# Expert tiles of 124 rows in place of 128, in a fused attention and mixture-of-experts kernel

## The reference

```python
def _moe_ref(x, w_gate, w_noise, noise, w1, w2):    # x 2304 x 512, 8 experts, w1 512 x 1024, w2 1024 x 512
    logits = x @ w_gate
    noisy_logits = logits + np.log1p(np.exp(x @ w_noise)) * noise
    top2 = np.argpartition(-noisy_logits, 2, axis=1)[:, :2]
    ...
    for e in range(E):
        for k in range(2):
            mask = top2[:, k] == e
            h = np.maximum(x[mask] @ w1[e], 0.0)
            out[mask] += top2_w[mask, k, None] * (h @ w2[e])
```

## Time and profile before

| | us |
|---|---|
| median of 3 runs | 809.34 |
| lowest and highest | 808.65, 811.51 |
| the profiled execution | 808.09 |
| its span, first to last instruction | 805.9 |
| TensorE busy in it | 764.0 (95%) |
| VectorE, ScalarE, GpSimd busy | 496.5, 391.5, 383.5 |

### The profile page before, as it was taken

One profiled execution on the slowest core, in us unless ns is written; L12 is line 12 of the kernel. 1 busy time (PEld: TensorE's weight loads), 2 busy tenths in 40 slices (PEclk: granted clock), 3 DMA queues, 4 the chain that ended last, 5 costly groups with the idle time before them and its releaser, 6 DMA issues.

```text
span 805.9 us, 18520 instructions
## 1 busy us (share of the span) xinstructions
PE 764.0 (95%) x6658; PEld 623.0 (77%) x6658; DVE 496.5 (62%) x1233; ACT 391.5 (49%) x835; POOL 383.5 (48%) x440
## 2 busy tenths in 40 slices
PE   4886999999999998998999999999999999999995
PEld 2345676776776665978898998998998988988984
DVE  5997999998998897875436235235344344353311
ACT  5995888888888776515324133233232232241200
POOL 0007999899899784055334324324414413423312
PEclk9997999999999999999999999999999999999998
DMA  7786343353353373228623714804804705714213
GB/s 161 215 235 138 107 133 103 104 163 105 105 160 103 88 223 132 69 53 289 192 111 66 205 71 75 242 24 78 261 6 77 257 13 82 245 26 65 41 22 44
DMA packets 51576, 98.49 MB, mean 122 GB/s; under 512 B 12721, under 2 KB 21553, under 8 KB 51505
## 3 DMA queue, kind: packets, MB, share of 16 engines
q1 hardware_dynamic: 39920, 74.55, 30.4%
q0 software_dynamic: 10720, 22.72, 14.9%
q10 hardware_dynamic: 864, 0.29, 0.2%
HBM read 66.38 MB, written 20.53 MB: 108 GB/s over the span
## 4 chain that ended last, share of the span: by engine, by line
PE 51%; DMA 3%; issue 1%; POOL 0%; POOLq 0%; ACT 0%; DVE 0%; ACTq 0%; DVEq 0%
PE ps L765 26%; PE po L779 23%; DMA out_rows<-ys,iscat 2%; PE pt L601 2%; DMA xg<-x_rows,rowi 1%; POOL out_rows L1585 0%; POOLq L163 0%; ACT xT L1458 0%; POOL wrow L1577 0%; DVE ys L1247 0%; ACTq L1490 0%; POOLq L1582 0%; POOLq L1585 0%; POOLq L1583 0%; POOLq L1584 0%
## 5 line engine op out<-in xcount | busy, mean ns | idle before, releaser
L765 PE MATMUL ps<-xT,whi 128*128 128x320 f32 (+1 forms) x960 | 164.1, 309 | 1.6 <-ACT xT L1458 1.6
L779 PE MATMUL po<-whi,hT 128*128 128x512 f32 x640 | 159.9, 395 | 0.0
L765 PEld LDWEIGHTS ps<-xT,whi 128*128 128x128 f32 x960 | 145.6, 189 | 2.6 <-issue 1.1
L1469 ACT ACTIVATE hT<-ps 128x320 fp32r<-128x320 f32 x112 | 49.0, 437 | 200.6 <-PE ps L765 200.6
L1232 DVE SCALAR_TENSOR_TENSOR hT<-ps,hT 128x320 fp32r<-128x320 f32 x112 | 55.1, 492 | 137.6 <-ACT hT L1469 137.6
L779 PEld LDWEIGHTS po<-whi,hT 128*128 128x128 f32 x640 | 118.3, 188 | 24.5 <-DVE hT L1077 0.5
L1532 POOL TENSOR_SCALAR work<-work,rcp 128x576 f32<-128x576 f32 (+1 forms) x160 | 117.6, 745 | 24.9 <-DVE rcp L947 24.1
L934 DVE CUSTOM_DVE_ANT_0 ns<-ps,slab 128x576 f32<-128x576 f32 (+1 forms) x160 | 119.8, 750 | 10.1 <-PE ps L595 6.3
L1324 ACT ACTIVATE work<-ns,nmax 128x576 f32<-128x576 f32 (+1 forms) x160 | 123.1, 769 | 4.4 <-DVE nmax L934 4.3
L1572 POOL DMA_INDIRECT xg<-x_rows,igath x38 | 42.3, 1112 | 168.7 <-DVE ys L1247 76.9
L1585 POOL DMA_INDIRECT out_rows<-ys,iscat x35 | 58.9, 1682 | 101.1 <-DMA out_rows<-ys,iscat 68.8
(11 more groups left out here) (184 smaller groups left out, 1111.0 us busy)
## 6 DMA issues: line engine op xcount, KB each, us to landing
wraw<-in_mw SPq DMA_DIRECT2D x64, 512.0 KB, 9.9
slab<-work SPq DMA_DIRECT2D x36, 288.0 KB, 3.8
qraw<-in_qT SPq DMA_DIRECT2D x64, 144.0 KB, 2.9
vs<-in_v SPq DMA_DIRECT2D x32, 160.0 KB, 2.5
out_rows<-zeros SPq DMA_DIRECT2D x32, 152.0 KB
kraw<-in_kT SPq DMA_DIRECT2D x64, 72.0 KB, 2.5
x_rows<-xnat SPq DMA_DIRECT2D x8, 576.0 KB, 4.2
xg<-x_rows,igath POOLq DMA_INDIRECT x38, 3.7
```

The lines of the kernel that those rows point to most:

```text
L765: mm = nc.tensor.matmul(ps[n % 4 // 2][:, n % 2, 0:w], w1s[i][pw][:, c, f * P:(f + 1) * P], x[px][:, c, :], start=j == 0 and c == 0, stop= ...
L779: mm = nc.tensor.matmul(po[:, (i + t) % 2, :], hT[px][:, c, t * P:(t + 1) * P], w2s[i][pw][:, c, :], start=j == 0 and c == 0, stop=j == 2 ...
```

## The change

A tile now holds ROWS = 124 rows and a block 620. Half a block is 310 columns; in the first block the halves are 372 and 248. Transposes, their copies, the indirect DMAs and the scaling work on 124 rows. The second layer still loads 128 columns of `hT` as its stationary operand, the last four of which belong to the next tile and give rows of `po` that nobody reads; `hT` is declared flat for it. Where there are no such columns (the last `c` of the last tile, and the third tile of the first block) it loads 124. The number of the tile is found by multiplying with 1/124 and rounding by adding and subtracting a large constant, the lane by subtracting 124 times the tile; `colv` holds tile numbers in place of multiples of 128. The thresholds of the block count are scaled by 124/128. Its core (the early forms `xtr0`, `xcopy0`, `xlow0`, `hhigh0`, `hlow0` and `scaled0`, and `xlow` and `weights`, change in the same way as those shown; `hC` takes the place of `hT` where ReLU and the low part are written):

```diff
@@ -49,14 +49,16 @@
-BLK = BT * P
+ROWS = P - 4
+BLK = BT * ROWS
 HB = BLK // 2
...
 XB = 3
 XLATE = {2: 3, 4: 4}
-HA = XB * P
+HA = XB * ROWS
+MAGIC = 1.5 * 2 ** 23
...
-            hT = [tmp(f"hT{i}", [P, CF, BLK], F32R) for i in range(2)]
+            hT = [tmp(f"hT{i}", [P, CF * BLK], F32R) for i in range(2)]
+            hC = [h[:, :].rearrange("p (c t) -> p c t", c=CF) for h in hT]
...
                 for c in range(CD):
-                    mm = tr(pt[i][:, c * P:(c + 1) * P], xg[t][:, c * P:(c + 1) * P], P)
+                    mm = tr(pt[i][:, c * ROWS:(c + 1) * ROWS], xg[t][0:ROWS, c * P:(c + 1) * P], ROWS)
                 mm.then_inc(xg_taken, 1)
...
-            def second(i, t, fresh=None):
+            def second(i, t, fresh=None, edge=False):
...
-                        mm = nc.tensor.matmul(po[:, (i + t) % 2, :], hT[px][:, c, t * P:(t + 1) * P],
+                        at, m = c * BLK + t * ROWS, ROWS if edge or (t == BT - 1 and c == CF - 1) else P
+                        mm = nc.tensor.matmul(po[0:m, (i + t) % 2, :], hT[px][:, at:at + m],
                                               w2s[i][pw][:, c, :],
...
-                second(0, t, CF if t == 0 else None)
+                second(0, t, CF if t == 0 else None, t == XB - 1)
...
+            def to_tile(which):
+                after(V.tensor_scalar(near[:, which], posk[:, which], 1.0 / ROWS, 0.5 / ROWS - 0.5, ALU.mult, ALU.add))
+                after(V.tensor_scalar(tileq[:, which], near[:, which], MAGIC, None, ALU.add))
+                after(V.tensor_scalar(hcol[:, which], tileq[:, which], -MAGIC, None, ALU.add))
+
+            def tile_and_lane(which):
+                to_tile(which)
+                after(V.scalar_tensor_tensor(out=lof[:, which], in0=hcol[:, which], scalar=float(-ROWS), in1=posk[:, which],
+                                             op0=ALU.mult, op1=ALU.add))
...
-            after(V.tensor_copy(poski[:, early], posk[:, early]))
-            after(V.tensor_scalar(loi[:, early], poski[:, early], P - 1, None, ALU.bitwise_and))
-            after(V.tensor_copy(lof[:, early], loi[:, early]))
-            after(V.tensor_tensor(hcol[:, early], posk[:, early], lof[:, early], ALU.subtract))
+            tile_and_lane(early)
...
-            after(V.tensor_tensor(over[:, :, :], inc[:, :, NT - 1:NT].broadcast_to([P, NE, NTHR]),
-                                  thr[:, 0:NT:BT].rearrange("p (a t) -> p a t", a=1).broadcast_to([P, NE, NTHR]),
-                                  ALU.is_gt))
+            after(V.scalar_tensor_tensor(out=over[:, :, :], in0=thr[:, 0:NT:BT].rearrange("p (a t) -> p a t", a=1)
+                                         .broadcast_to([P, NE, NTHR]), scalar=ROWS / P,
+                                         in1=inc[:, :, NT - 1:NT].broadcast_to([P, NE, NTHR]),
+                                         op0=ALU.mult, op1=ALU.is_lt))
...
-            after(V.tensor_copy(poski[:, :], posk[:, :]))
-            after(V.tensor_scalar(loi[:, :], poski[:, :], P - 1, None, ALU.bitwise_and))
-            after(V.tensor_copy(lof[:, :], loi[:, :]))
-            after(V.tensor_tensor(hcol[:, :], posk[:, :], lof[:, :], ALU.subtract))
+            tile_and_lane(slice(0, 2 * NT))
...
-                    V.tensor_scalar(ys[(i + t) % 2][:, :], po[:, (i + t) % 2, :], wrow[:, t, bass.ds(e, 1)], None, ALU.mult)\
+                    V.tensor_scalar(ys[(i + t) % 2][0:ROWS, :], po[0:ROWS, (i + t) % 2, :], wrow[0:ROWS, t, bass.ds(e, 1)], None, ALU.mult)\
                         .then_inc(y_done, 1)
...
-                nc.scalar.activation(xT[0][:, :, t * P:(t + 1) * P], pt[i][:, :].rearrange("p (c t) -> p c t", c=CD),
+                nc.scalar.activation(xT[0][:, :, t * ROWS:(t + 1) * ROWS],
+                                     pt[i][:, 0:CD * ROWS].rearrange("p (c t) -> p c t", c=CD),
                                      ACT.Copy).then_inc(xhi_done, 1)
...
-                nc.gpsimd.tensor_scalar(colv[:, :], iota[:, 0:NL], float(P), None, ALU.mult).then_inc(consts_done, 1)
+                nc.gpsimd.tensor_copy(colv[:, :], iota[:, 0:NL]).then_inc(consts_done, 1)
...
-                nc.gpsimd.indirect_dma_start(out=xg[t][:, :], out_offset=None, in_=xs[0:n, :],
-                                             in_offset=bass.IndirectOffsetOnAxis(ap=rows, axis=0),
+                nc.gpsimd.indirect_dma_start(out=xg[t][0:ROWS, :], out_offset=None, in_=xs[0:n, :],
+                                             in_offset=bass.IndirectOffsetOnAxis(ap=rows[0:ROWS], axis=0),
...
-                nc.gpsimd.indirect_dma_start(out=out, out_offset=bass.IndirectOffsetOnAxis(ap=index, axis=0),
-                                             in_=ys[i][:, :], in_offset=None, compute_op=ALU.add,
+                nc.gpsimd.indirect_dma_start(out=out, out_offset=bass.IndirectOffsetOnAxis(ap=index[0:ROWS], axis=0),
+                                             in_=ys[i][0:ROWS, :], in_offset=None, compute_op=ALU.add,
```

More of the change, by code:

```diff
@@ L276, in build @@
         posk = cut([P, 2 * NT])
-        poski = cut([P, 2 * NT], I32)
-        loi = cut([P, 2 * NT], I32)
+        near = cut([P, 2 * NT])
+        tileq = cut([P, 2 * NT])
         over = cut([P, NE, len(range(0, NT, BT))])
@@ L750, in xtr0 @@
                 for c in range(CD):
-                    mm = tr(dst[:, c * P:(c + 1) * P], xg[t][:, c * P:(c + 1) * P], P)
+                    mm = tr(dst[:, c * ROWS:(c + 1) * ROWS], xg[t][0:ROWS, c * P:(c + 1) * P], ROWS)
                 mm.then_inc(xg_taken, 1)
@@ L1076, in hlow0 @@
                 dve.wait_ge(hhi_done, n + 1)
-                V.scalar_tensor_tensor(out=hT[1][:, f, cols], in0=ps[n % 4 // 2][:, n % 2, 0:cols.stop - cols.start], scalar=0.0,
-                                       in1=hT[0][:, f, cols].bitcast(F32), op0=ALU.max, op1=ALU.subtract)\
+                V.scalar_tensor_tensor(out=hC[1][:, f, cols], in0=ps[n % 4 // 2][:, n % 2, 0:cols.stop - cols.start], scalar=0.0,
+                                       in1=hC[0][:, f, cols].bitcast(F32), op0=ALU.max, op1=ALU.subtract)\
                     .then_inc(hlo_done, 1)
@@ L1084, in scaled0 @@
                 dve.wait_ge(y_added, C_ADD + 16 * (t - 1))
-                V.tensor_scalar(ys[t % 2][:, :], po[:, t % 2, :], wrow[:, t, 0:1], None, ALU.mult).then_inc(y_done, 1)
+                V.tensor_scalar(ys[t % 2][0:ROWS, :], po[0:ROWS, t % 2, :], wrow[0:ROWS, t, 0:1], None, ALU.mult).then_inc(y_done, 1)
             evac0(TILES - 7)
@@ L1221, in xlow @@
                 dve.wait_ge(xhi_done, g + 1)
-                cols = slice(t * P, (t + 1) * P)
-                V.tensor_tensor(xT[1][:, :, cols], pt[i][:, :].rearrange("p (c t) -> p c t", c=CD),
+                cols = slice(t * ROWS, (t + 1) * ROWS)
+                V.tensor_tensor(xT[1][:, :, cols], pt[i][:, 0:CD * ROWS].rearrange("p (c t) -> p c t", c=CD),
                                 xT[0][:, :, cols].bitcast(F32), ALU.subtract).then_inc(xlo_done, 1)
@@ L1231, in block_of @@
                     dve.wait_ge(hhi_done, C_HALVES * b + n + 1)
-                    V.scalar_tensor_tensor(out=hT[1][:, f, cols], in0=ps[n % 4 // 2][:, n % 2, 0:HB], scalar=0.0,
-                                           in1=hT[0][:, f, cols].bitcast(F32), op0=ALU.max, op1=ALU.subtract)\
+                    V.scalar_tensor_tensor(out=hC[1][:, f, cols], in0=ps[n % 4 // 2][:, n % 2, 0:HB], scalar=0.0,
+                                           in1=hC[0][:, f, cols].bitcast(F32), op0=ALU.max, op1=ALU.subtract)\
                         .then_inc(hlo_done, 1)
@@ L1399, in xcopy0 @@
                 act.wait_ge(xg_taken, t + 1)
-                nc.scalar.activation(xTa[0][:, :, t * P:(t + 1) * P], src.rearrange("p (c t) -> p c t", c=CD),
+                nc.scalar.activation(xTa[0][:, :, t * ROWS:(t + 1) * ROWS],
+                                     src[:, 0:CD * ROWS].rearrange("p (c t) -> p c t", c=CD),
                                      ACT.Copy).then_inc(xhi_done, 1)
@@ L1406, in hhigh0 @@
                 act.wait_ge(h_ready, n + 1)
-                nc.scalar.activation(hT[0][:, f, cols], ps[n % 4 // 2][:, n % 2, 0:cols.stop - cols.start], ACT.Relu)\
+                nc.scalar.activation(hC[0][:, f, cols], ps[n % 4 // 2][:, n % 2, 0:cols.stop - cols.start], ACT.Relu)\
                     .then_inc(hhi_done, 1)
@@ L1412, in scaled0 @@
                 act.wait_ge(w_rows, 16 * XB)
-                nc.scalar.activation(ys[t % 2][:, :], po[:, t % 2, :], ACT.Copy, scale=wrow[:, t, 0:1]).then_inc(y_done, 1)
+                nc.scalar.activation(ys[t % 2][0:ROWS, :], po[0:ROWS, t % 2, :], ACT.Copy, scale=wrow[0:ROWS, t, 0:1]).then_inc(y_done, 1)
             evac1(TILES - 5)
@@ L1468, in block_of @@
                     act.wait_ge(h_ready, C_HALVES * b + n + 1)
-                    nc.scalar.activation(hT[0][:, f, half * HB:(half + 1) * HB], ps[n % 4 // 2][:, n % 2, 0:HB], ACT.Relu)\
```

(9 more changed lines are left out.)

4 lines of the change are left out of this document (2 added, 2 removed).

## The result

The changed kernel takes 940.32 us (median of 4 runs, 938.26 to 942.38), the one before 809.0 beside it: a ratio of 1.1617, 95% interval 1.1593 to 1.164. It is 131 us slower. The profiled execution has a span of 936.1 us.

What follows compares the result with a forecast made beforehand. TensorE was taken to bound the kernel until the last block, where the scatter chain sets the end. Terms of -5.6, -0.3 and -0.2 plus -0.2 from bounds gave -6.3 us: median 803.0, own range 800.5 to 805.5, with rivals 793.5 to 810.5.

Steps and rivals of the forecast that it cites:

- gathers, row weights and scatters: Indirect DMAs of 124 rows: only the last block's scatters on the path, slightly shorter, -0.2 us.
- rival A: Transfers of 124 rows run on 4 DMA engines; scatter pitch 11.9 us, total about 915 us; chance 0.14.
- First layer, 310 columns: In seven blocks 1344 matmuls lose 10 columns, 4.17 ns each, with a fixed part of 13.4 ns: -5.6 us.
- B: Rival: matmuls of 310, 372 and 248 columns cost what the old sizes did; median 809.1 us; chance 0.10.
- C: Rival: the first-layer matmuls' fixed part falls to that at 256 columns; median 794 us; chance 0.08.
- D: Rival: shifted starts raise the matmuls' fixed part, or 48 short loads are laid bare; median 807 to 816; chance 0.06.
- First block: Matmuls shrink from 384 to 372 and 256 to 248 columns; only the second lot on the path: -0.3 us.
- Second layer at 0: 960 matmuls with 512 moving columns of w2 keep 229.6 ns each: 0 us.
- 124-column loads at 0: 48 second-layer matmuls load 124 columns, hidden behind their neighbours: 0 us, at most 9.0 us if bare.
- Routing, ReLU and low parts: Small DVE routing operations and slightly shorter scalar and vector work: 0 us; routing at worst 0.1 us.
- transposes: 40 tiles of four transposes with 124 rows, probably set by their load: 0 us, -0.5 as a bound.
- 8 blocks: Every expert's rows fit in 620, so the loop still runs eight blocks.

Runs made afterwards that it cites:

- e7: The kernel before with only the scatters cut to 124 of a tile's 128 rows: one run of 933.54 us beside 807.88.
- e2: e1 with only the gathers at 124 rows, row weights and scatters staying at 128: 818.24 us, ratio 1.0104.
- e3: The changed kernel with only the gathers at 128 rows, row weights and scatters staying at 124: 935.24 us, ratio 1.1555.
- e9: e1 with scatters of 125 rows: one run of 889.54 us.
- e1: The changed kernel with gathers, row weights, scaling and scatters on all 128 rows, the last four padding: 806.47 us against 809.83, ratio 0.9962.
- e5: The kernel before with hT and xT (and three tiles of xg) starting 16 bytes later: one run of 811.84 us beside 807.88.
- e8: The kernel before, tiles and DMAs still 128 rows, but 620 rows counted per block, 108 in the last tile: 805.05 us against 807.88, ratio 0.9966.

## Why the prediction was wrong

**The step that failed** is the one on gathers, row weights and scatters, which priced 124 rows in proportion to 128 (-0.2 us) and held that only the scatters of the last block are on the path, and the 0.14 given to rival A beside it. A is what happened: the scatter pitch rose from 5.86 to 11.3 us, and scatters set the time of every block. The Trainium skill's rule stood in that very step, and the sum went against it without a row that spoke for its own reading: the trace had one shape, and could not tell a share that follows the rows from one that follows the divisors. e7 shows that this step is nearly the whole result: 126 of 131 us.

**A's own working** was right in kind and mostly in size. The 8.1 us of data that it put in place of 2.1 were a little over 7 (windows above); the pitch of 11.9 was 11.3; the tail's +30 was +27.2; +14 us a block was (445.4 - 354.8) / 6 = 15.1. It missed the first gathers and scatters, +12.4 us ahead of block 1 (e2, e3). It took the gain of 6 us off beside the 14 a block, though a block that waits for its scatters can't show it. It counted every scatter at the pitch of the tail, where the third of a block took up to 16.11 us. Its limit in the loop, the row weights of the next block, is the one that ended last. But it is not the only one: the profile shows a second a few us behind, DVE's queue, in which the last `ys`, waiting for the third scatter, holds up the low parts that TensorE needs some 7 us into the next block; by the times before that is at 450 + 7 = 429.7 + 3S, so again from about 9 us on. In e9, whose scatters are shorter and whose row weights have 128 rows, DVE scales the first tile without a wait for them, and this second limit sets the block alone. 808.1 + 12.4 + 90.6 + 27.2 is the 938.3 of the profiled execution; A had said 915.

**First layer, 310 columns: right.** 18.83 us for 132, 142.7 ns, a gain of 4.0 ns where 4.17 was forecast; the fixed part stayed at 13.5 ns. Rivals B and C are out. So is the part of D that blamed the start at 1240 bytes: e1's first and second halves take 1.71 and 1.70 us for 12.

**First block: partly wrong.** In e1 12 matmuls of 372 columns take 2.04 us and 12 of 248 columns 1.37 us, where 256 columns took 1.36 before:

```profile
335.98 1.52 PE L768 MATMUL ps<-xTa,whi 128*128 128x372 f32 x8
...
338.02 1.52 PE L768 MATMUL ps<-xTa,whi 128*128 128x372 f32 x8
...
371.43 0.62 PE L768 MATMUL ps<-xT,wlo 128*128 128x248 f32 x4
...
372.80 0.62 PE L768 MATMUL ps<-xT,wlo 128*128 128x248 f32 x4
```

The 8 columns less brought nothing: 0.3 us counted, 0 found. A fixed part of 6.6 ns belongs to 256 columns, and isn't had at 248.

**Second layer at 0: wrong by a little.** 5.56 for 5.51 us, about 2 ns on each of 960, 0.25 us a block. The prediction named the starts at multiples of 496 bytes under D and priced them from the first layer's side; e5 shows that the stationary operand is the one that minds. Six such layers ahead of the last block's first scatter are 1.5 us, the first block 0.3, the scatters 0.2: with them 6.3 becomes 4.3, and e1's profiled execution shows 3.9, its ratio 1.9 to 4.4.

**124-column loads at 0: not separated** in e1, where they stand beside the shifted starts; e8 shows 4 to 5 ns for loads of 108. **Routing, ReLU and low parts, transposes, 8 blocks**: nothing of them shows on the chain, as forecast; the transposes take 0.43 us for four in place of 0.44.

## What to carry to other kernels

Keep the outer dimension of a DMA at 128, or at a count with a large divisor up to 16; take rows off what is computed, and let the transfer move padding. Four rows fewer took the landing of a scatter from 5.0 to 10.4 us; two fewer cost 0.3 us of pitch. When a trace shows one shape only, a rule that is about shape can't be discounted by that trace; a run with a single transfer changed would have told.

A chain of transfers, each waiting for the one before, has a slack that can be estimated from the trace of before: here a mean pitch of about 9 us by POOL's fetch of the weights and by DVE's written order alike. It has to be held against the pitch in the loop, not in the tail: e9 has 9.7 us in the tail, but its third scatter takes 15.17 beside the weight load, and its first block in the loop took 493.86 - 425.28 = 68.6 us, 11.3 more than in e1. If the price of a change lies beyond the slack, it is multiplied by the number of blocks.

## What the runs showed of the hardware

- An accumulating scatter of n rows by a list of indices had 144, 160, 416 and 512 packets for n of 128, 126, 125 and 124, the counts of 16, 14, 5 and 4 DMA engines. A gather had 80 and 272 for 128 and 124, the counts of 16 and 4. Landing of a scatter: 5.0 us at 128, 10.4 at 124.
- TensorE's granted clock fell to 0.50 during a wait of 13.22 us, and 12 matmuls of 310 columns behind it took 3.44 us in place of 1.71.
- In fp32r with a load for each matmul, moving `hT` and `xT` by 16 bytes put 3.8 ns on each matmul of 512 columns, 0.5 us a block, and nothing on those of 320. A load of 108 columns in place of 128 put 4 to 5 ns on it.
- 248 moving columns took 114 ns, and 256 took 113.
